# Attention and two MLPs on one core: one projection stretch in place of two, and the seventh product moved behind the next step's second

## The reference

```python
def reference(q, k, v, w1, w2, w3, w_out, w2_in, w2_out):
    # q, k, v: 8 batches x 8 heads x 576 x 64; keys and values are pooled by 8 (mean) to 72
    attn = softmax(q @ pooled_k.T / sqrt(64)) @ pooled_v        # 4608 tokens x 512
    x2 = maximum(maximum(attn @ w1, attn @ w2), attn @ w3) @ w_out   # d_ff 768
    h = x2 @ w2_in                                              # 512 -> 2048
    g = h - tanh(h)
    return g @ w2_out                                           # 2048 -> 512
```

## Time and profile before

| | |
|---|---|
| median of 3 runs | 1440.73 us (1439.23 to 1441.86) |
| profiled execution, time | 1439.83 us |
| profiled execution, span | 1438.0 us |
| TensorE busy | 1424.2 us (99%) |
| VectorE busy | 1006.7 us (70%) |
| ScalarE busy | 653.8 us (45%) |
| granted TensorE clock | full (1.00) |

### The profile page before, as it was taken

One profiled execution on the slowest core, in us unless ns is written; L12 is line 12 of the kernel. 1 busy time (PEld: TensorE's weight loads), 2 busy tenths in 40 slices (PEclk: granted clock), 3 DMA queues, 4 the chain that ended last, 5 costly groups with the idle time before them and its releaser, 6 DMA issues.

```text
span 1438.0 us, 26270 instructions
## 1 busy us (share of the span) xinstructions
PE 1424.2 (99%) x10794; PEld 1236.1 (86%) x10794; DVE 1006.7 (70%) x1765; ACT 653.8 (45%) x1291; POOL 96.4 (7%) x140
## 2 busy tenths in 40 slices
PE   8899999999999999999999999999999999999998
PEld 7888888888888878788899999999999999999997
DVE  7786666665656555534887777777777777777777
ACT  3322222222222221223676665666666566665655
POOL 2302121212121100000000000000000000000000
PEclk9999999999999999999999999999999999999999
DMA  6544444443534211155977666676766667676551
GB/s 224 200 148 138 167 142 166 143 165 127 180 128 152 99 60 60 52 198 208 326 271 256 220 234 228 214 254 219 254 220 225 235 218 256 213 250 223 194 184 52
DMA packets 81335, 269.74 MB, mean 188 GB/s; under 512 B 7168, under 2 KB 21504, under 8 KB 69568
## 3 DMA queue, kind: packets, MB, share of 16 engines
q1 hardware_dynamic: 81216, 268.07, 54.0%
HBM read 210.89 MB, written 57.15 MB: 186 GB/s over the span
## 4 chain that ended last, share of the span: by engine, by line
PE 95%; DVE 2%; DMA 2%; ACT 0%; issue 0%; SPq 0%; DVEq 0%; ACTq 0%
PE psum L676 29%; PE psum L716 27%; PE psum L740 25%; PE psum L690 10%; PE psum L619 2%; PE psum L659 2%; DMA v_first<-in_v 0%; DMA w_raw<-in_w 0%; DMA w_mid_raw<-in_w_mid 0%; DVE probs L1059 0%; DMA k_first<-in_k 0%; DMA k_raw<-in_k 0%; PE psum L803 0%; DVE h L1091 0%; PE psum L698 0%
## 5 line engine op out<-in xcount | busy, mean ns | idle before, releaser
L676 PE MATMUL psum<-x,w 128*128 128x512 f32 (+1 forms) x2160 | 452.7, 370 | 5.8 <-ACT first_copy L844 3.1
L676 PEld LDWEIGHTS psum<-x,w 128*128 128x128 f32 x2160 | 375.7, 188 | 77.1 <-ACT first_copy L844 3.3
L716 PE MATMUL psum<-w_out_s,g 128*128 128x512 f32 x1668 | 404.7, 391 | 0.5 <-DVE g L1126 0.4
L716 PEld LDWEIGHTS psum<-w_out_s,g 128*128 128x128 f32 x1668 | 304.3, 188 | 58.8 <-DVE g L1126 1.4
L740 PEld LDWEIGHTS psum<-x_even,ring 128*128 128x128 f32 x1680 | 212.7, 191 | 6.5
L740 PE MATMUL psum<-x_even,ring 128*128 128x256 f32 x1680 | 215.0, 283 | 0.0
L1131 DVE SCALAR_TENSOR_TENSOR poly<-poly,u_sq 128x512 f32<-128x512 f32 x144 | 99.0, 688 | 141.1 <-ACT poly L896 141.1
L740 PEld LDWEIGHTS psum<-x_odd,ring 128*128 128x128 f32 x1344 | 170.0, 191 | 5.0
L740 PE MATMUL psum<-x_odd,ring 128*128 128x256 f32 x1344 | 171.9, 283 | 0.0
L852 ACT ACTIVATE h<-best 128x512 fp32r<-128x512 f32 (+1 forms) x60 | 35.4, 589 | 276.1 <-DVE best L1085 276.1
L690 PE MATMUL psum<-h,w_mid_s 128*128 128x512 f32 x648 | 152.3, 391 | 0.0
(11 more groups left out here) (82 smaller groups left out, 1085.8 us busy)
## 6 DMA issues: line engine op xcount, KB each, us to landing
ring<-w_scratch SPq DMA_DIRECT2D x72, 1024.0 KB, 5.1
ring<-w_scratch SPq DMA_DIRECT2D x72, 768.0 KB, 4.4
x_scratch<-x_stage SPq DMA_DIRECT2D x18, 1024.0 KB, 4.2
x_odd<-x_scratch SPq DMA_DIRECT2D x28, 512.0 KB, 5.5
x_even<-x_scratch SPq DMA_DIRECT2D x28, 512.0 KB, 5.5
x_scratch<-x_stage SPq DMA_DIRECT2D x18, 768.0 KB, 3.4
w_scratch<-w_stage SPq DMA_DIRECT2D x32, 384.0 KB, 2.6
v_raw<-in_v SPq DMA_DIRECT2D x21, 512.0 KB, 4.6
```

What stands on the lines that cost most here:

```text
L676: mm = pe.matmul(psum[:, bank, 0:hi - lo], w123[:, m, ws, n, c, :], x[:, xs, c, lo:hi], start=(c == 0 and ws + xs == 0), stop=(c == KC1 - ...
L716: mm = pe.matmul(psum[:, j, :], g_of(c)[:, gs, j * P:(j + 1) * P], w_out_s[:, row_of(c), ws, :], start=(m == 0 and gs + ws == 0), stop=(m ...
```

## The change

TensorE's step becomes: product 0, product 1, product 6 of the step before (`last_product(s - 1)`), products 3 and 2, 24 projection matmuls (both chunks), products 4 and 5. Product 6 has semaphores of its own (`last_multiplied`, `last_copied`), so `multiplied` counts six and `copied` four to a step. In step 71 only one chunk is projected inside; the other and the last product 6 follow the loop. ScalarE copies the first two products at the head of its step and only then takes product 6 of the step before; VectorE moves `sum_first` and the low parts of g ahead and `sum_third` ahead of the second `choose`. SP issues half 1 of the ring one product later, in the next step, ahead of `load_x2`, and `store_out` ahead of it. `drain_out` and `piece_high` stay where they are written, behind `copy_sum(s, 2)`.

```diff
@@ SP step
+                if t > 0 and p == 2:
+                    store_out(t - 1)
+                if s > 0 and s + 1 < ALL2:
+                    sp.wait_ge(last_multiplied, s)
+                    load_w((p + 1) % STEPS2, 1)
                 if 0 < t < NT - 1 and p < PRODUCTS:
                     load_x2(t + 1, p)
-                if t > 0 and p == 2:
-                    store_out(t - 1)
                 if s + 2 < ALL2:
-                    sp.wait_ge(multiplied, PRODUCTS * s + 4)
+                    sp.wait_ge(multiplied, 6 * s + 4)
                     load_w((p + 2) % STEPS2, 0)
...
-                if s + 2 < ALL2:
-                    sp.wait_ge(multiplied, PRODUCTS * s + PRODUCTS)
-                    load_w((p + 2) % STEPS2, 1)
@@ TensorE
-            def between(s, n):
+            def between(s):
                 if s < EARLY:
-                    layer2(("l2", NT - 1, C_ORDER[s + 1]), range(3 * n, 3 * n + 3))
+                    layer2(("l2", NT - 1, C_ORDER[s + 1]))
                 else:
-                    project(2 * (s - 2) + n, range(SUB))
+                    project(2 * (s - 2), range(SUB))
+                    if s < ALL2 - 1:
+                        project(2 * (s - 2) + 1, range(SUB))
+            def last_product(s):
+                pe.wait_ge(copied, 4 * s + 4)
+                multiply(s, 6, main_banks(s)[0], False, True).then_inc(last_multiplied, 1)
...
                 if s >= 2:
-                    pe.wait_ge(copied, 5 * s - 5)
-                multiply(0, main, True, False)
+                    pe.wait_ge(last_copied, s - 1)
+                multiply(s, 0, main, True, False).then_inc(multiplied, 1)
                 if s >= 1:
                     pe.wait_ge(summed, 3 * s - 2)
-                multiply(1, second, True, False)
-                between(s, 0)
-                pe.wait_ge(copied, 5 * s + 1)
-                multiply(3, main, False, False)
+                multiply(s, 1, second, True, False).then_inc(multiplied, 1)
+                if s >= 1:
+                    last_product(s - 1)
+                pe.wait_ge(copied, 4 * s + 1)
+                multiply(s, 3, main, False, False).then_inc(multiplied, 1)
                 if s >= 1:
                     pe.wait_ge(summed, 3 * s - 1)
-                multiply(2, third, True, True)
+                multiply(s, 2, third, True, True).then_inc(multiplied, 1)
+                between(s)
                 pe.wait_ge(w_in_half[p % 2][1], 16 * loads)
-                pe.wait_ge(copied, 5 * s + 2)
-                multiply(4, second, False, True)
-                pe.wait_ge(copied, 5 * s + 3)
-                multiply(5, main, False, False)
-                between(s, 1)
-                pe.wait_ge(copied, 5 * s + 4)
-                multiply(6, main, False, True)
+                pe.wait_ge(copied, 4 * s + 2)
+                multiply(s, 4, second, False, True).then_inc(multiplied, 1)
+                pe.wait_ge(copied, 4 * s + 3)
+                multiply(s, 5, main, False, False).then_inc(multiplied, 1)
@@ behind the loop over the steps
+            project(2 * ALL2 - 5, range(SUB))
+            last_product(ALL2 - 1)
@@ ScalarE step
+                act.wait_ge(multiplied, 6 * s + 1)
+                if s > 0:
+                    act.wait_ge(summed, 3 * s - 2)
+                copy_sum(s, 0)
+                act.wait_ge(multiplied, 6 * s + 2)
+                if s > 0:
+                    act.wait_ge(summed, 3 * s)
+                copy_sum(s, 3)
+                if s > 1:
+                    g_hi(c - 1, 1)
                 if s > 0:
                     copy_last(s - 1)
                     square(s - 1, 0)
                     shifted_square(c, 0, 0)
+                act.wait_ge(multiplied, 6 * s + 3)
+                copy_sum(s, 1)
+                if s > 0:
                     tanh(s - 1, 0)
-                if s > 1:
-                    g_hi(c - 1, 1)
-                act.wait_ge(multiplied, PRODUCTS * s + 1)
-                copy_sum(s, 0)
-                act.wait_ge(multiplied, PRODUCTS * s + 2)
-                if s > 0:
-                    act.wait_ge(summed, 3 * s)
-                copy_sum(s, 3)
...
                     tanh(s - 1, 1)
-                act.wait_ge(multiplied, PRODUCTS * s + 3)
-                copy_sum(s, 1)
-                if s > 0:
                     shifted_square(c + 1, 1, 1)
                     g_hi(c, 0)
-                act.wait_ge(multiplied, PRODUCTS * s + 6)
+                act.wait_ge(multiplied, 6 * s + 6)
                 copy_sum(s, 2)
                 if t > 0 and p == 1:
                     drain_out(t - 1, range(SUB))
@@ VectorE step
+                if s > 1:
+                    g_lo(c - 1, 1)
+                sum_first(s)
                 if s > 0:
                     small_part(c, 0, 0)
                     mask(s - 1, 0)
                     both_parts(c, s - 1, 0, 0)
-                if s > 1:
-                    g_lo(c - 1, 1)
-                if s > 0:
                     choose(c, s - 1, 0, 0)
                 if s == 1:
                     x2_sums_low(NT - 1, 0)
-                sum_first(s)
...
                     mask(s - 1, 1)
+                    g_lo(c, 0)
                 sum_second(s)
                 if s == 2:
                     x2_sums(("l2", NT - 1, C_ORDER[3]))
                 if s > 0:
-                    g_lo(c, 0)
                     both_parts(c + 1, s - 1, 1, 1)
+                sum_third(s)
+                if s > 0:
                     choose(c + 1, s - 1, 1, 1)
-                sum_third(s)
@@ VectorE tail
             s, c = ALL2 - 1, 2 * ALL2 - 2
+            dve.wait_ge(h_drained, c)
```

More of the change, by code:

```diff
@@ L345, in fused_attention_mlps @@
         multiplied = sem("multiplied")
+        last_multiplied = sem("last_multiplied")
         copied = sem("copied")
+        last_copied = sem("last_copied")
         summed = sem("summed")
@@ L721, in project, with multiply @@
                     mm.then_inc(steps_projected, 1)
-            def between(s, n):
+            def between(s):
                 if s < EARLY:
-                    layer2(("l2", NT - 1, C_ORDER[s + 1]), range(3 * n, 3 * n + 3))
+                    layer2(("l2", NT - 1, C_ORDER[s + 1]))
                 else:
-                    project(2 * (s - 2) + n, range(SUB))
+                    project(2 * (s - 2), range(SUB))
+                    if s < ALL2 - 1:
+                        project(2 * (s - 2) + 1, range(SUB))
+            def multiply(s, n, bank, fresh, whole):
+                t, p = s // STEPS2, s % STEPS2
+                for j in range(KHALF):
+                    for ws, xs in split_passes():
+                        mm = pe.matmul(psum[:, bank, 0:HALF], ring[:, p % 2, n, j, ws], x2[t % 2][:, j, X_OF[n], xs],
+                                       start=(fresh and j + ws + xs == 0), stop=(j == KHALF - 1 and ws == 1),
+                                       skip_group_check=not (fresh and whole))
+                return mm
+            def last_product(s):
+                pe.wait_ge(copied, 4 * s + 4)
+                multiply(s, 6, main_banks(s)[0], False, True).then_inc(last_multiplied, 1)
             def step(s):
@@ L734, in step @@
                 loads = STEPS2 // 2 * t + p // 2 + 1
[L736 to L743, removed]
                 if p == 0:
@@ L902, in copy_last @@
             def copy_last(s):
-                act.wait_ge(multiplied, PRODUCTS * s + PRODUCTS)
+                act.wait_ge(last_multiplied, s + 1)
                 act.wait_ge(summed, 3 * s + 1)
-                nc.scalar.activation(h2[:, s % 2, 0, HALF:TB], psum[:, main_banks(s)[0], 0:HALF], ACT.Copy).then_inc(copied, 1)
-                act.wait_ge(copied, 5 * s + 5)
+                nc.scalar.activation(h2[:, s % 2, 0, HALF:TB], psum[:, main_banks(s)[0], 0:HALF], ACT.Copy)\
+                    .then_inc(last_copied, 1)
+                act.wait_ge(last_copied, s + 1)
             def drain_out(t, js):
@@ L1149, in sum_first @@
             def sum_first(s):
-                dve.wait_ge(multiplied, PRODUCTS * s + 4)
-                dve.wait_ge(copied, 5 * s + 1)
+                dve.wait_ge(multiplied, 6 * s + 4)
+                dve.wait_ge(copied, 4 * s + 1)
                 nc.vector.tensor_tensor(h2[:, s % 2, 0, 0:HALF], psum[:, main_banks(s)[2], 0:HALF], copies[:, 0], ALU.add)\
@@ L1155, in sum_second @@
             def sum_second(s):
-                dve.wait_ge(multiplied, PRODUCTS * s + 5)
-                dve.wait_ge(copied, 5 * s + 3)
+                dve.wait_ge(multiplied, 6 * s + 5)
+                dve.wait_ge(copied, 4 * s + 3)
                 nc.vector.tensor_tensor(h2[:, s % 2, 1, 0:HALF], psum[:, main_banks(s)[1], 0:HALF], copies[:, 1], ALU.add)\
@@ L1161, in sum_third @@
             def sum_third(s):
-                dve.wait_ge(copied, 5 * s + 4)
+                dve.wait_ge(copied, 4 * s + 4)
```

## The result

The changed kernel takes 1445.24 us (median of 6 runs, 1444.21 to 1448.09) against 1440.53 (6 runs, 1437.2 to 1441.86) for the kernel before on the same chip: ratio 1.0040 between the means of these runs, 95% interval 1.0026 to 1.0055 (the two medians alone give 1.0033). It is slower by 0.40%. The forecast was 1446.5 us, slower by 0.40%, within 1438.8 to 1451.

The account below looks back on a forecast made before the run. The prediction took TensorE's own work, busy 99% of the span, as the bound. Terms 6.2 + 1.3 - 1.4 - 0.1 - 0.2 gave +5.8 us on 1440.7, so 1446.5 us, 8-in-10 range 1438.8 to 1451.

Parts of the forecast that it names:

- The drains: ScalarE, step p = 1 of tiles 1 to 8: four drains delay copy_sum 0, product 3 stalls 0.77 us eight times, +6.2 us.
- The joints: TensorE, one projection stretch in place of two: 0.02 us saved a step over 68 steps, -1.4 us (0 to -2.7).
- first_project: Start of stage 2, once: its second half waits for x2_sums on VectorE, +1.3 us (0 to 2.5).
- Ordinary steps: Steps without drains: every copy and sum ready before TensorE needs it, no cost, 10.50 us a step.
- The 1 us of slack: VectorE in an ordinary step: sum_second can start at 9.95 when product 4 is done, VectorE's preceding work over at 9.0.
- The tail: End of stage 2: sum_third of the last step ahead of choose, at hand earlier, -0.2 us (+0.5 to -0.5).
- The DMAs: SP's ring load of half 1 moves into the next step, late w_out pieces go ahead of one ring load: costed at nothing.
- the joints in the steps with layer 2: The three steps that carry layer 2: one stretch in place of two adds -0.1 us.
- The upper end of the forecast's own range: Slower by the drain stalls, chance 0.72: 1442.7 to 1453, upper bounds 10.1 + 2.5 + 0.5 and no gain.
- hidden drains: Rival: ScalarE reaches copy_sum 0 by T+1.6, so product 3 doesn't wait; 1439 to 1440.3 us, chance 0.13.
- a wait in every step: Rival: VectorE's round exceeds 10.5 us, each step waits 0.2, 13 us on top, 1460 us, chance 0.08.
- dearer joints: Rival: joints give the whole 0.04, the tail 0.5, stalls at lower ends: +2.0, 1442.7 us, chance 0.03.

Follow-up runs that it names:

- Experiments 1 and 2: Changed kernel with all four drains ahead of copy_sum(s, 2): 1439.82 us, ratio 0.9998; with three left behind it 1443.76 us, with two behind 1440.64 us.
- experiment 4: Changed kernel with the drains ahead of copy_sum(s, 2) and its 24 projection matmuls cut in three stretches in steps 3 to 70: 1443.99 us, one run.
- Experiment 3: Changed kernel with the drains ahead of copy_sum(s, 2) and step 2's last x2 chunk ahead on ScalarE and VectorE: 1438.18 us, ratio 0.9988.
- experiment 5: Changed kernel with VectorE's order of before put back as a whole: 1651.05 us, one run.
- experiment 6: Changed kernel with VectorE's order of before but g_lo(c - 1, 1) first: 1453.07 us; changed kernel with only g_lo(c - 1, 1) late: 1527.40 us.

## Why the prediction was right

**The drains.** Forecast 0.77 us eight times, 6.2 in all; measured 0.81 (11.31 against 10.50), 6.5. The place, the order and the starts on ScalarE were right to 0.01 us. The 0.04 missing is the length of the copy behind the drains, 0.43 where a single copy takes 0.38; this is the one term of the stall that was mis-sized. The row of another line, four copies of the same width out of PSUM, priced the drains: 0.48 apart there, 0.48 here (1023.27 to 1025.18). The figure worked out from the Trainium skill (ScalarE: Activation LUTs, section "What ACT_TABLE_LOAD costs"), 0.52, is an estimate and would have made the stall 0.17 longer; the traces of both kernels disagree with it for sources in PSUM. Experiments 1 and 2 show the cause by taking it away and by changing its dose.

**The joints.** Forecast 0.02 us each, measured 0.02 from both sides (experiment 4). 68 x 0.02 is -1.4. The formula of the Trainium skill that the prediction quotes (TensorE: Matmul & The Clock Gate, section "Back-to-back issue gap") has no such term, and the steps of 10.50, 10.52 and 10.54 show one. The page calls that formula the gap of an isolated matmul and says that in a stream with weight loads the spacing is set by both; the prediction left this out when it read it as holding "whatever stands before it".

**first_project.** Forecast 1.3, measured 1.3 (6.80 - 5.46), by the same bank and the same sum: step 2 begins at 678.93, the bank was forecast free 13.0 us later, and the second half starts at 692.05, 13.1 later. Experiment 3 removes the wait.

**Ordinary steps.** Forecast free, and so they are: 10.50 in all that have no drain, those with piece_high among them. The 1 us of slack is in the trace of the kernel after as well. Without the longest wait, which is in step 0, `sum_second` waits for product 4 65.3 us in 67 steps, 0.97 each:

```profile
DVE h L1171 <- PE psum L740: 69.7, 68, 4.4
```

Experiments 5 and 6 show how near the edge lay: one VectorE instruction, a few places later in its queue, makes every step 1.2 us longer. The forecast checked g's low part against the moment at which it is wanted (3.5 against 6.3); it is that line which carried the change, not the busy share.

**Step 0.** Product 3's wait of 0.06 us wasn't in the forecast; the same copy had been looked at for ordinary steps only, where product 6 stands between.

**The tail.** Forecast -0.2, measured -0.25. From the last product to the last 12 matmuls it is 1431.49 - 1421.41 = 10.08 us before and 1435.68 - 1425.85 = 9.83 after. The last product is the first row in the kernel before and the second in the kernel after:

```profile
1421.41 0.88 PE L740 MATMUL psum<-x_even,ring 128*128 128x256 f32 x6
...
1425.85 0.88 PE L740 MATMUL psum<-x_even,ring 128*128 128x256 f32 x6
```

Only the first of the two waits became shorter.

**The DMAs.** Forecast nothing, and no matmul or weight load of stage 2 waits for one in the kernel after.

**The sum.** The terms as measured, 6.46 + 1.33 - 1.36 + 0.06 - 0.25, and -0.07 for the joints in the steps with layer 2, make the 6.17 us by which stage 2 grew. The forecast was 5.8; 4.7 lies between the medians and 5.8 between the means. That forecast and ratio agree to the last digit, 0.40%, is luck within an interval of 0.26% to 0.55%; the terms are what was right. The upper end of the forecast's own range is added up wrongly: 10.1 + 2.5 + 0.5 on 1440.7 is 1453.8, not 1453, which changes nothing here. The rivals: hidden drains are refuted by the eight waits, a wait in every step by 10.50, and dearer joints by 0.02.

## What to carry to other kernels

When matmuls are moved ahead, look at each engine's queue between the new wait and its release: work that was free behind a copy (here four drains of 0.48 us) becomes a stall as soon as the next copy in that queue has a matmul waiting. Price such a stall by counting starts from a row of the same shape and source, not by durations, and take the loop of waits over all engines, TensorE too, before calling an order free. A change that reads as a loss of 0.4% may hold a gain of 0.1% and two misplaced pieces of work, as here: move them before dropping the change.

## What the runs showed of the hardware

**The clock fell after some waits of 1.9 us.** In experiment 5 this is the view of three stretches (length, busy time and count of each engine, then granted clock):

```profile
1000.00:1002.20 2.20, 0.30 (x3) 0.04 (x1) 2.20 (x5) 1.07 (x3) 0.00 (x0) 1.00 1.04 390
1002.20:1006.60 4.40, 4.40 (x12) 3.45 (x13) 1.80 (x4) 1.25 (x2) 0.00 (x0) 0.61 0.31 131
1006.60:1016.40 9.80, 8.21 (x55) 7.15 (x53) 6.12 (x12) 6.98 (x15) 0.00 (x0) 1.00 0.65 216
```

TensorE was busy for 0.30 of the first 2.2 us; most of the next 12 matmuls then ran at the lower level, 1.2 GHz, and cost 1.6 us on top of the wait. TensorE had stood idle for 1.90 us before them. The 1.09 us before 1016.44 had no such effect, nor had the 0.9 us in each step of the kernel with the low part late. In the tail of the other kernel of experiment 6 the clock fell too, to 0.57 on average from 1438 to 1442 us, after 1.95 us idle. In experiment 5's trace TensorE stood idle for 1.9 to 2.0 us 59 times; the 12 matmuls behind took 4.3 to 4.5 us in 36 cases and 2.9 in the other 23. So the wait alone doesn't decide it; what does stays open.

**Copies in a row grow longer, but start as evenly.** The four drains of 512 columns lasted 0.59, 0.60, 0.62 and 0.63 us and began 0.48 us apart. The copy of 256 columns behind them lasted 0.43 us instead of 0.38; behind three drains it was 0.42, behind two 0.41. Whoever waits for the end of the last one pays for it.
